# Attention on one core: the transposes of the probabilities as two row tiles of 64 queries, the rest product and the output rows as two column tiles

## What is computed

```python
# attention: batch 4, heads 8, sequence 576, head size 64
scores = scale * q @ k.T
thresh = max(scores, -1) - tau
scores = where(scores >= thresh, scores, -1e9)
attn = exp(scores - max(scores, -1))
attn = attn / (sum(attn, -1) + 1e-9)
x = attn @ v                      # then heads side by side: 2304 x 512
# experts: the one with the largest logit, weighted with its softmax share
logits = x @ w_gate + modality_bias[modality_id]
out[mask] = gate_w[mask] * (relu(x[mask] @ w1[e]) @ w2[e])
# last layer
h = x @ w_in;  out = (h * tanh(softplus(h))) @ w_out
```

## Time and profile before

| | us |
|---|---|
| median of three runs | 978.95 |
| lowest and highest | 978.39 and 979.11 |
| the profiled execution, its time | 979.82 |
| the profiled execution, its span | 978.1 |
| TensorE busy in the span | 953.1 |
| VectorE, ScalarE, GpSimd busy | 676.4, 512.4, 477.8 |

### The profile page before, as it was taken

How to read it: one execution, slowest core, us unless ns; L and a number is a source line. 1 busy time by engine, 2 the same in 40 slices (tenths; PEclk the granted TensorE clock), 3 DMA queues, 4 the chain that set the end, 5 groups by cost and what they waited for, 6 DMA issues and landing times.

```text
span 978.1 us, 17785 instructions
## 1 busy us (share of the span) xinstructions
PE 953.1 (97%) x6144; PEld 797.4 (82%) x6145; DVE 676.4 (69%) x1227; ACT 512.4 (52%) x987; POOL 477.8 (49%) x560
## 2 busy tenths in 40 slices
PE   7999999999999999999999998999999999999997
PEld 5777777777778878888887887888989889889995
DVE  6888888888885541111134499878888878888793
ACT  5666676767764232222244465555555555555452
POOL 4222225555441266200000087786786787777784
PEclk9999999999999999999999999999999999999999
DMA  3122128224121656211216200100100100000000
GB/s 126 51 73 74 50 73 304 83 73 128 50 71 32 194 182 225 67 46 46 77 46 237 80 0 1 33 34 1 33 33 1 33 33 1 22 12 1 33 1 33
DMA packets 21930, 65.86 MB, mean 67 GB/s; under 512 B 3552, under 2 KB 3552, under 8 KB 21600
## 3 DMA queue, kind: packets, MB, share of 16 engines
q1 hardware_dynamic: 14512, 39.90, 12.0%
q0 software_dynamic: 4896, 20.00, 6.0%
q10 hardware_dynamic: 2448, 5.01, 1.8%
HBM read 46.63 MB, written 18.27 MB: 66 GB/s over the span
## 4 chain that ended last, share of the span: by engine, by line
PE 63%; DVE 5%; issue 4%; ACT 1%; ACTq 0%; POOL 0%; DVEq 0%; POOLq 0%
PE psum L1356 6%; PE psum L1358 6%; PE psum L1357 6%; PE psum L1348 6%; PE psum L1346 6%; PE psum L1347 6%; PE psum L1019 3%; PE psum L1021 3%; PE psum L1020 3%; PE psum L1046 3%; PE psum L1048 3%; PE psum L1047 3%; DVE rr L1468 2%; PE psum L1030 2%; PE psum L440 1%
## 5 line engine op out<-in xcount | busy, mean ns | idle before, releaser
L1468 DVE RECIPROCAL rr<-rr 128x384 f32<-128x384 f32 x96 | 244.1, 2543 | 10.0 <-ACT rr L1416 10.0
L523 ACT ACTIVATE prob<-ssb,smin 128x576 f32<-128x576 f32 x144 | 111.6, 776 | 77.5 <-DVE ssb L642 77.5
L1294 POOL TENSOR_TENSOR uu<-uu,ex 128x384 f32<-128x384 f32 x96 | 97.4, 1015 | 100.5 <-ACT uu L1410 100.5
L642 DVE TENSOR_SCALAR_CACHE_REDUCE ssb<-psum,tauk 128x576 f32<-128x576 f32 x144 | 112.5, 814 | 41.8 <-PE psum L399 41.4
L1346 PE MATMUL psum<-x2T_hi,w_in_hi 128*128 128x384 f32 x384 | 131.2, 342 | 4.3 <-DVE gg L1474 2.7
L1348 PE MATMUL psum<-x2T_hi,w_in_lo 128*128 128x384 f32 x384 | 129.7, 338 | 0.0
L1347 PE MATMUL psum<-x2T_lo,w_in_hi 128*128 128x384 f32 x384 | 129.1, 336 | 0.0
L316 POOL TENSOR_TENSOR limit<-smin,margin 128x2 f32<-128x2 f32 (+1 forms) x80 | 57.6, 720 | 145.9 <-DVE ssb L642 145.5
L1100 DVE TENSOR_TENSOR hT_lo<-psum,hT_hi 128x512 fp32r<-128x512 f32 x38 | 26.3, 691 | 141.2 <-ACT hT_hi L1077 135.8
L1356 PE MATMUL psum<-w_hi,g_hi 128*128 128x512 f32 x288 | 114.3, 397 | 0.1
L1358 PE MATMUL psum<-w_hi,g_lo 128*128 128x512 f32 x288 | 114.0, 396 | 0.0
(11 more groups left out here) (206 smaller groups left out, 2208.4 us busy)
## 6 DMA issues: line engine op xcount, KB each, us to landing
qk<-in_qk_dram SPq DMA_DIRECT2D x15, 640.0 KB, 4.1
vsb<-in_v_dram SPq DMA_DIRECT2D x16, 512.0 KB, 3.5
xrow<-xs ACTq DMA_DIRECT2D x17, 288.0 KB, 2.9
ys<-ysb SPq DMA_DIRECT2D x19, 257.0 KB, 3.2
stage<-in_w_in_dram POOLq DMA_DIRECT2D x16, 256.0 KB, 4.2
wa<-in_wa_dram SPq DMA_DIRECT2D x8, 512.0 KB, 6.8
wb<-in_wb_dram SPq DMA_DIRECT2D x8, 512.0 KB, 10.6
xs<-zrow SPq DMA_DIRECT2D x11, 288.0 KB, 3.2
```

The source lines that it names most:

```text
L523: act.activation(prob[:, n % 3, cols], ssb[:, w, cols], ACT.Exp, bias=smin[:, w, h:h + 1], scale=-1.0).then_inc(exp_done, 1)
L642: dve.tensor_scalar(ssb[:, w, h * S:(h + 1) * S].rearrange("p (a q) -> p a q", a=2), banks(n)[h], factor, BIG, ALU.mult, ALU.min, accum_ou ...
L1468: dve.reciprocal(rr[:, n % 4], rr[:, n % 4]).then_inc(r_done, 1)
```

## The change

`turn` handles tiles with n % 5 other than 1 in another way (`by_half`): each transpose of a block of 128 queries x 128 keys becomes two, one for queries 0 to 63 on array rows 0 to 63, one for queries 64 to 127 on array rows 64 to 127. The weights of such a half are 64 rows x 128 columns and its moving operand is 64 columns of the identity. The near halves go to one bank and the far halves to another. A far half has nine blocks in a full tile and a bank takes eight, so the first far block of a full tile goes to the rest bank, and the last near block too. For this the wait for `ot_out` is moved to the head of `turn` in those tiles, and a new semaphore `far_turned` stands before the last near block. The last tile of a pair doesn't write the rest bank and has no wait for `ot_out`. Tiles with n % 5 equal to 1 keep the whole transposes and their order. In all, the wait for `rest_out` goes to the head.

`pv` issues the block of the rests as two column tiles, and `rows_out` its products as two column tiles too. The evacuation copies as many columns as before, with a layout in two halves (`pt` holds the near halves first and the far halves 576 columns further on), which `pv` reads as 2 x 64 columns.

```diff
+    FAR = S
+    def by_half(n):
+        return n % TT != 1
+    def halved(n):
+        return 3 * (n // TT) + n % TT + 1 - (n % TT > 0)
+    def both_halves(w, first, cols, apart):
+        base = pt[:, w, first:first + cols]
+        return bass.AP(base.tensor, base.offset, [list(base.ap[0]), [apart, 2], [1, cols]])
+    def turned_block(n, b):
+        w = n % 2
+        if not by_half(n):
+            return pt[:, w, b * P:(b + 1) * P]
+        return both_halves(w, b * D, D, FAR)
...
+            if n >= 1:
+                pe.wait_ge(rest_out, n)
+            blocks = QT if not full else 2 * QT
+            def other_bank():
+                if n >= 2:
+                    pe.wait_ge(ot_out, min(n - 1, NS - 3))
+            if by_half(n):
+                def half_block(place, h, b):
+                    rows = slice(h * D, h * D + D)
+                    key = b * P if b < QT else (S + REM + (b - QT) * P if b < 2 * QT else QT * P)
+                    return pe.transpose(place, prob[rows, w, key:key + P], ident[rows, rows])
+                if full:
+                    other_bank()
+                    half_block(rest_bank[:, D:2 * D], 1, 0).then_inc(far_turned, 1)
+                else:
+                    half_block(turn_bank[:, 1, 0:D], 1, 0)
+                half_block(turn_bank[:, 0, 0:D], 0, 0)
+                for b in range(1, blocks):
+                    if b == QT:
+                        pe.wait_ge(prob_done, units(n + 1))
+                    at = b - full
+                    half_block(turn_bank[:, 1, at * D:at * D + D], 1, b)
+                    half_block(turn_bank[:, 0, b * D:b * D + D], 0, b)
+                at = blocks - full
+                half_block(turn_bank[:, 1, at * D:at * D + D], 1, 2 * QT)
+                if full:
+                    pe.wait_ge(far_turned, halved(n))
+                    half_block(rest_bank[:, 0:D], 0, 2 * QT).then_inc(turned, 1)
+                else:
+                    half_block(turn_bank[:, 0, QT * D:QT * D + D], 0, 2 * QT).then_inc(turned, 1)
+                return
...
-                pe.matmul(ot, vsb[:, u, VBD:VBD + P], pt[:, w, 2 * QT * P:],
-                          start=False, stop=True).then_inc(pv_done, 1)
+                for h in range(2):
+                    last = pe.matmul(ot[h * D:(h + 1) * D, :], vsb[:, u, VBD + h * D:VBD + (h + 1) * D],
+                                     turned_block(n, 2 * QT), start=False, stop=True)
+                last.then_inc(pv_done, 1)
...
-            last = pe.matmul(row_bank[:, c:c + 2 * HW], otsb[:, n % 2],
-                             wx[:, p % HP].rearrange("p h c -> p (h c)"), start=True, stop=True)
+            for h in range(2):
+                rows = slice(h * D, h * D + D)
+                last = pe.matmul(row_bank[rows, c:c + 2 * HW], otsb[:, n % 2, rows],
+                                 wx[:, p % HP].rearrange("p h c -> p (h c)"), start=True, stop=True)
...
-                act.copy(pt[:, w, 2 * QT * P:], rest_bank).then_inc(rest_out, 1)
-                act.copy(pt[:, w, 0:2 * QT * P], turn_bank.rearrange("p a q -> p (a q)")).then_inc(main_out, 1)
+                act.copy(pt[:, w, QT * P:QT * P + P], rest_bank).then_inc(rest_out, 1)
+                act.copy(both_halves(w, 0, QT * P, QT * P + P), turn_bank).then_inc(main_out, 1)
```

More of the change, by code:

```diff
@@ L182, in attention_phase @@
     turned = sem("turned")
+    far_turned = sem("far_turned")
     main_out = sem("main_out")
@@ L423, in turn @@
+            for j in range(QT):
+                pe.transpose(turn_bank[:, 1, j * P:(j + 1) * P],
+                             prob[:, w, S + REM + j * P:S + REM + (j + 1) * P], ident[:])
+            other_bank()
             pe.transpose(rest_bank, prob[:, w, QT * P:QT * P + P], ident[:]).then_inc(turned, 1)
@@ L440, in pv @@
                         pe.matmul(ot[h * D:(h + 1) * D, :], vsb[:, u, (h * QT + j) * D:(h * QT + j + 1) * D],
-                                  pt[:, w, (h * QT + j) * P:(h * QT + j + 1) * P], start=(j == 0), stop=False)
-                pe.matmul(ot, vsb[:, u, VBD:VBD + P], pt[:, w, 2 * QT * P:],
-                          start=False, stop=True).then_inc(pv_done, 1)
+                                  turned_block(n, h * QT + j), start=(j == 0), stop=False)
+                for h in range(2):
+                    last = pe.matmul(ot[h * D:(h + 1) * D, :], vsb[:, u, VBD + h * D:VBD + (h + 1) * D],
+                                     turned_block(n, 2 * QT), start=False, stop=True)
+                last.then_inc(pv_done, 1)
             else:
@@ L448, in pv @@
                             v = vsb[:, u, VTURN + j * D:VTURN + (j + 1) * D] if h else vsb[:, u, j * D:(j + 1) * D]
-                            pr = pt[:, w, j * P + h * D:j * P + (h + 1) * D]
+                            pr = pt[:, w, h * FAR + j * D:h * FAR + (j + 1) * D]
                         else:
                             v = vsb[:, u, VREST + h * D:VREST + (h + 1) * D]
-                            pr = pt[:, w, 2 * QT * P + h * D:2 * QT * P + (h + 1) * D]
+                            pr = pt[:, w, h * FAR + QT * D:h * FAR + (QT + 1) * D]
                         last = pe.matmul(ot[h * D:(h + 1) * D, 0:REM], v, pr, start=(j == 0), stop=(j == QT))
@@ L467, in rows_out @@
             c = (tt % 2) * 2 * HW
-            last = pe.matmul(row_bank[:, c:c + 2 * HW], otsb[:, n % 2],
-                             wx[:, p % HP].rearrange("p h c -> p (h c)"), start=True, stop=True)
+            for h in range(2):
+                rows = slice(h * D, h * D + D)
+                last = pe.matmul(row_bank[rows, c:c + 2 * HW], otsb[:, n % 2, rows],
+                                 wx[:, p % HP].rearrange("p h c -> p (h c)"), start=True, stop=True)
             if tt == QT:
                 pe.wait_ge(summed, norms(n + 1))
-                last = pe.matmul(moved, t["shift"], rsum[:, p % 2, 2 * QT:TPP], start=True, stop=True)
+                for h in range(2):
+                    rows = slice(h * D, h * D + D)
+                    last = pe.matmul(moved[rows], t["shift"][:, rows], rsum[:, p % 2, 2 * QT:TPP], start=True, stop=True)
             last.then_inc(rows_done, 1)
@@ L530, in evacuate @@
                 act.wait_ge(pv_done, n - 1)
-            if n % TT < QT:
+            if not by_half(n):
                 act.copy(pt[:, w, 2 * QT * P:], rest_bank).then_inc(rest_out, 1)
                 act.copy(pt[:, w, 0:2 * QT * P], turn_bank.rearrange("p a q -> p (a q)")).then_inc(main_out, 1)
-            else:
-                act.copy(pt[0:REM, w, 2 * QT * P:], rest_bank[0:REM, :]).then_inc(rest_out, 1)
-                act.copy(pt[:, w, 0:QT * P], turn_bank[:, 0, :]).then_inc(main_out, 1)
+            elif n % TT < QT:
+                act.copy(pt[:, w, QT * P:QT * P + P], rest_bank).then_inc(rest_out, 1)
+                act.copy(both_halves(w, 0, QT * P, QT * P + P), turn_bank).then_inc(main_out, 1)
+            else:
+                act.copy(both_halves(w, QT * D, D, FAR), turn_bank[:, :, QT * D:QT * D + D]).then_inc(rest_out, 1)
+                act.copy(both_halves(w, 0, QT * D, FAR), turn_bank[:, :, 0:QT * D]).then_inc(main_out, 1)
         def copy_out(n):
```

## The result

The change makes the kernel slower by less than forecast: 985.88 us in the median of five runs (984.85 to 986.74) against 979.11 for the kernel before on the same chip; the ratio is 1.0066, its 95% interval 1.0051 to 1.0081. That is +6.8 us where 15.6 were forecast: the sign and the place held, the size didn't, and a part of the loss has other reasons than the forecast's.

The account below looks back on a forecast made before the run. TensorE was taken to bound the kernel, busy 953.1 of 978.1 us; 11.3 + 4.1 + 0.2 = 15.6 us more gave a span of 993.7 and a median of 994.5, own range 986 to 1004, with rivals 974 to 1008.

Parts of the forecast that it names:

- The wait at the head: Before the first half transpose in n % 5 = 0, 2, 3: 0.54 us of waiting, such a step 0.25 us longer.
- The price of a pair: Two half transposes loading side by side on TensorE: 0.107 us a pair, the same as a whole transpose.
- 45 x 0.25 = 11.3: Loss in us over the 45 turns from n = 2 to 75 that wait at the head, 0.25 us each.
- the halves are cheap: Rival at the nine pairs behind the wait: 0.055 us a pair, 975.6 us; decides from 0.064 downwards; chance 0.12.
- Late copies: In 13 of the 45 steps extra VectorE work delays the copy; their excess above 0.25 sums to 4.1 us.
- The last tile of a pair: Turn of n % 5 = 4: 0.26 us gained, all given back because VectorE is next in line; net 0.
- 15 x 0.26 = 3.9 us of gain: What the last tiles of pairs (n % 5 = 4) would gain if VectorE had room there.
- Shapes: Array shape changes in a full step fall from three to two, saving 0.17 to 0.2 us if nothing else holds it.
- No change beyond 0.01: Rest product and rows as column tiles: 0.21 and 0.24 us, where the whole passes took 0.22 and 0.23.
- Tiles with n % 5 = 1: Whole transposes, wait at the end as before; a pause before them replaces the one before the rows: 0.
- moving the wait for `rest_out`: In turn: the wait is for a copy ScalarE does ahead of one already waited for; cost 0.
- the 0.2 for n = 77: The turn of n = 77, near the end of attention, adds 0.2 us.

Follow-up runs that it names:

- the head wait: Kernel before, whole transposes kept, with only the wait for ot_out moved to the head of turn in the same 45 turns: 1006.11 us, ratio 1.027.
- column tiles alone: Kernel before with the rest product and output rows as two column tiles, transposes whole and their waits as before: 977.02 us, ratio 0.9977.
- six pairs ahead: Changed kernel with the bank 6 far block and the wait for ot_out moved back behind six pairs of halves: 973.68 us, ratio 0.9937.
- the last tile only: Changed kernel with halves only where n % 5 = 4, whole transposes in other full tiles with their wait at the end: 971.43 us, ratio 0.9919.
- the mix: Changed kernel with halves for n % 5 = 3 (six pairs before the ot_out wait) and 4, other tiles whole, wait at end: 968.55 us, ratio 0.9884.
- fillers: Changed kernel with twenty extra near halves before the wait for ot_out in turns n = 30, 47, 50, 67 and 70: 983.71 us, ratio 1.0045.

## Why the prediction was wrong in its size, point by point

**The wait at the head: right, place and mechanism.** TensorE stands idle before the halves in the named classes, 37.3 us in 42 waits, released by the copy, first load 0.11 behind it. The run with the wait alone gives the term's working back within 0.02 us a step.

**The price of a pair: the step that failed.** The prediction put it as "What binds is the load" and took 0.107. It is 0.062. That the halves of a pair load side by side was right; that each costs a plain product's load was not, and the agreement with 0.107 to 0.12 that the prediction names is one of plain products' loads and of whole transposes. From the end of the copy to the next scores it is 0.66 instead of 1.01, so the term "45 x 0.25 = 11.3" is 45 x (0.25 - 0.35) = -4.5, and the sum of 15.6 us falls to about 0. The measured cycles agree with the sign (18.13 for 18.36). The price sits at the point of decision that the rival "the halves are cheap" named, 0.064, nearer to its 0.055 than to the forecast. The error was to price a transpose's load by a plain product's (line 472), when 64 rows by 128 columns of a transpose load every 0.062 us.

**What fills the gap between about 0 and 6.8.** The two profiled executions differ by 5.3 us of span, and their step times, from scores to scores, come apart like this. The ordinary change of each class gives -3.4 us. Steps 33, 50 and 70, with the clock falls, lie 3.7 above their classes; the forecast had no such term. Steps with a late copy lie 6.2 above theirs, the ranks below included. The first five steps give 0.3. Steps 34, 53, 73 and 76 give -1.4, of which 0.55 is a stall of the kernel before in step 76 (4.00 us, where the runs with the head wait and with column tiles alone have 3.45). The clock's share of the medians stays open: in the five executions of the change the mean granted clock is 0.986 to 0.994 (0.996 to 0.999 in those of the kernel before), but the time doesn't follow it, 984.85 us at 0.989 and 985.06 at 0.994.

In steps 32, 52 and 72 the rank products (lines 537 and 538, whole array) stand between the halves and the scores: in the timeline after,

```profile
122.48 0.24 ACT L606 COPY otsb<-psum 128x128 f32<-128x128 f32 x1
122.84 0.67 PEld L448 LDWEIGHTS psum<-ident,prob 64*128 64x128 f32 x18 [1.65 <-issue]
...
123.57 0.30 PEld L537 LDWEIGHTS psum<-oh,ltri 128*128 128x128 f32 x2
...
124.15 0.18 PEld L419 LDWEIGHTS psum<-qk 64*128 64x128 f32 x1
```

the next scores are 1.43 behind the copy's end and not 0.66: the ranks add 0.77, where before they added 0.32 (0.63 from line 423's load to the scores, for 0.31 in other steps). They now stand between two row tile parts, two changes of shape more; 3 x 0.45 = 1.4 us of the 6.2. That is read, not tried.

**Late copies: right in kind.** Class 2 and 4 steps with extra VectorE work lose more than the ordinary ones (step 27: 4.54 for 3.85, step 49: 5.23 for 4.84). Over all such steps the excess above the ordinary ones is 6.2 - 1.4 = 4.8 us, where the forecast had 4.1. Some of it comes back in the step behind (step 53: 3.55 for 4.08).

**The last tile of a pair: right in outcome, wrong in reason.** Classes 1 and 2 together are 7.17 for 7.29 before, so the 0.45 that class 1 gains is mostly given back. The prediction laid that to VectorE alone ("VectorE takes the scores only when it is free"). The run with halves in that tile only shows that VectorE's lateness has room under a wait at the end, and that the head wait is what passes it on. Its "15 x 0.26 = 3.9 us of gain" was there to be had, and more: that run is 5.6 us under the one with column tiles alone.

**Shapes: right about the pause, wrong about one neighbour.** The pause moved from before the rest product to before the transposes (0.20 before line 448 or 471 where no copy is awaited), and the saved one is worth nothing beside the wait. "No change beyond 0.01" for rest product and rows left out the shift product, and the column tiles alone gain 2.4 us.

**Tiles with n % 5 = 1, and what lies behind attention: nearly right.** Class 3 is 3.13 for 3.17. The forecast put moving the wait for `rest_out` at 0; with it gone from before the last whole transpose, that load starts 0.05 us behind the copy's end and not 0.11. The scores of step 79 are 5.4 us later and the span ends 5.3 later, so attention's loss passes through as a whole, and the 0.2 for n = 77 doesn't show.

## What to carry to other kernels

A wait belongs before the one instruction that needs it; before moving it to the head of a group, follow the released engine's own chain back, and if it begins at work that stands behind the wait, the loop closes and everything in it is paid each time (27 us here). A price for an instruction must come from a row of its own kind: a transpose's load and a plain product's load of as many columns differed in recorded length (0.14 and 0.18 us). The pitch of a stream says only what its slowest part costs, and its mean can mix two parts: 0.052 was neither the pitch on one tile nor that on two. Where a change brings new idle time of TensorE, look at the granted clock of the stretches behind the longest waits.

## What the runs showed of the hardware that wasn't expected

- Half transposes (64 rows x 128 columns loaded, 64 columns moved): 0.062 us each on one row tile, and 0.062 a pair where both tiles run; whole ones 0.107. Their loads, recorded with 0.14 us each, follow one another on one tile every 0.062.
- The granted clock fell to 0.63 to 0.65 in the mean of single steps behind TensorE waits of 1.4 to 1.9 us, in places that differ between kernels and executions. Not every such wait did it: in the run with the head wait and whole transposes the longest wait was 1.5 us, and the stretch from 20 to 320 us is at 1.00 in the mean; in the change it stayed up behind the longest, 2.0 us.
- A half that waits for the completion of one issued five places ahead of it came 0.20 us later than its place in the stream (load 0.33 for 0.13 behind the first, with six pairs ahead).
- From the end of ScalarE's copy to the load that waited for it, it is 0.11 us in over 40 waits each of the kernel before, of the change's halves and of the head wait, and 0.05 in over 30 each with six pairs ahead, with the last tile only and in the mix, and in the 14 of the change's whole transposes. Where it is 0.11, another wait of TensorE stands directly before the one for `ot_out`; where it is 0.05, a transpose does. In the run with fillers both occur in one execution: 0.05 in the five turns with fillers, 0.11 in the rest. It fits in every run and was not tried by itself.
